# Every product of the two up layers as a pair of 64-row matmuls, with the inputs on both halves of the partitions

## The reference, cut to what matters

```python
x = attn_out.reshape(B * S, D)            # 8192 x 192: out[s] = sum_k w[head, k] * x[s - 6 + k]
g = x @ w_gate                            # 192 -> 1536
val = x @ w_val                           # 192 -> 1536
y = (g / (1 + exp(-g)) * val) @ w_out1    # 1536 -> 192
h = y @ w_in2                             # 192 -> 2048
a = where(h > 0, h, exp(min(h, 0)) - 1)
out = a @ w_out2                          # 2048 -> 192
```

## Time and profile before

| | |
|---|---|
| median of 2 runs | 1329.24 us (1328.96 to 1329.53) |
| profiled execution | 1330.26 us, span 1328.5 us |
| PE busy | 1314.7 us (99%), 6240 matmuls |
| DVE, ACT, POOL busy | 797.7, 667.7, 653.8 us |
| granted TensorE clock, mean | 0.997 |

### The profile page before, as it was taken

The page is one execution under the profiler, slowest core; times in us unless marked ns, Lnnn a source line. Parts: engine busy times, 40 slices in busy tenths (PEclk is TensorE's granted clock), DMA queues, the critical chain, the costliest instruction groups (busy, mean ns, idle before and its releaser), DMA issues.

```text
span 1328.5 us, 19686 instructions
## 1 busy us (share of the span) xinstructions
PE 1314.7 (99%) x6240; PEld 1036.9 (78%) x6240; DVE 797.7 (60%) x1196; ACT 667.7 (50%) x1104; POOL 653.8 (49%) x477
## 2 busy tenths in 40 slices
PE   7999999999999999999999999999999999999998
PEld 5768778687786877878788787877878778687787
DVE  7667466564665646557555675556656456564675
ACT  5455545454453644545455454554535545354454
POOL 5574445454454544545445454454544445454454
PEclk8999999999999999999999999999999999999999
DMA  8221000010010100101001010100001000010000
GB/s 186 54 74 25 13 9 16 12 24 12 8 17 11 24 12 8 28 0 24 12 11 24 0 24 12 22 13 8 16 12 24 12 8 16 12 24 12 8 13 13
DMA packets 93858, 28.15 MB, mean 21 GB/s; under 512 B 77456, under 2 KB 90256, under 8 KB 93840
## 3 DMA queue, kind: packets, MB, share of 16 engines
q1 hardware_dynamic: 93840, 27.93, 9.4%
HBM read 17.43 MB, written 6.29 MB: 18 GB/s over the span
## 4 chain that ended last, share of the span: by engine, by line
PE 96%; DVE 2%; issue 1%; ACT 0%; POOL 0%; POOLq 0%; DVEq 0%; ACTq 0%
PE up L769 55%; PE down L769 41%; DVE mixed L742 1%; DVE mixed L576 0%; DVE hidden L634 0%; ACT act L498 0%; DVE act L673 0%; DVE hidden L692 0%; DVE out_w L296 0%; ACT out_w L289 0%; DVE in_a_lo L582 0%; POOLq L67 0%; DVE hidden L735 0%; POOL hid_lo L384 0%; POOL head_of L368 0%
## 5 line engine op out<-in xcount | busy, mean ns | idle before, releaser
L384 POOL TENSOR_TENSOR hid_lo<-hidden,hid_hi 128x512 fp32r<-128x512 f32 x447 | 628.8, 1407 | 661.5 <-ACT hid_hi L480 387.0
L634 DVE TENSOR_TENSOR hidden<-act,up 128x512 f32<-128x512 f32 x192 | 131.8, 687 | 310.4 <-ACT act L467 307.2
L519 ACT ACTIVATE hid_hi<-hidden 128x512 fp32r<-128x512 f32 x256 | 162.0, 633 | 208.9 <-DVE hidden L692 208.9
L692 DVE SCALAR_TENSOR_TENSOR hidden<-act,up 128x512 f32<-128x512 f32 x256 | 175.7, 686 | 121.7 <-ACT act L498 117.3
L467 ACT ACTIVATE act<-up 128x512 f32<-128x512 f32 x192 | 114.7, 598 | 231.1 <-PE up L769 230.8
L769 PE MATMUL down<-out_w,hid_hi 128*128 128x384 f32 x1024 | 225.8, 342 | 0.3 <-DVE result L619 0.2
L673 DVE TENSOR_SCALAR act<-up 128x512 f32<-128x512 f32 x256 | 176.4, 689 | 63.2 <-PE up L769 57.9
L769 PEld LDWEIGHTS down<-out_w,hid_hi 128*128 128x128 f32 x1024 | 184.6, 188 | 28.5 <-issue 7.3
L480 ACT ACTIVATE hid_hi<-hidden 128x512 fp32r<-128x512 f32 x192 | 121.5, 633 | 162.2 <-PE down L769 91.2
L498 ACT ACTIVATE act<-act 128x512 f32<-128x512 f32 x256 | 161.2, 630 | 45.1 <-DVE act L673 39.0
L769 PE MATMUL down<-hid_hi,out_w 128*128 128x512 f32 x576 | 182.1, 424 | 0.0
(11 more groups left out here) (141 smaller groups left out, 1792.1 us busy)
## 6 DMA issues: line engine op xcount, KB each, us to landing
x_raw<-x_dram SPq DMA_DIRECT2D x144, 64.0 KB, 2.2
out_dram<-result SPq DMA_DIRECT2D x15, 384.0 KB, 2.6
swapped<-halves SPq DMA_DIRECT2D x32, 128.0 KB, 2.3
stage<-w_out_dram SPq DMA_DIRECT2D x7, 384.0 KB, 3.5
stage<-w_in_dram SPq DMA_DIRECT2D x4, 256.0 KB, 2.9
stage<-w_in_dram SPq DMA_DIRECT2D x8, 128.0 KB, 2.9
stage<-w_gate_dram SPq DMA_DIRECT2D x4, 192.0 KB, 4.2
stage<-w_val_dram SPq DMA_DIRECT2D x4, 192.0 KB, 4.6
```

The costliest lines, as they stand in the source:

```text
L384: return pool.tensor_tensor(hid_lo[:, slot, :], hidden[:, s, :], hid_hi[:, slot, :].bitcast(F32), ALU.subtract)
L519: nc.scalar.activation(hid_hi[:, k % RING, :], hidden[:, k % 2, :], ACT.Copy)\
L634: v.tensor_tensor(hidden[:, f % 2, :], act[:, f % 2, :], val_bank(f)[:, :], ALU.mult)\
L692: v.scalar_tensor_tensor(hidden[:, k % 2, :], act[:, k % 2, :], -1.0, elu_bank(n, k)[:, :], ALU.add, ALU.max).then_inc(elu_done, 1)
```

## The change

All up products of both layers are done as pairs of 64-row matmuls. The 192 channels are three groups of 64, and the weights of a group lie for two different blocks on the two halves: gate above and val below in the first layer, blocks 2j and 2j + 1 in the second. Nine pairs (three groups x three products) make two blocks. The data must lie on both halves: slot MAIN holds channels 0 to 63 above and 64 to 127 below, CROSSED the same with halves exchanged, written by DMA from MAIN, and TWICE the tail on both. In MAIN the upper half works on group 0 while the lower works on group 1, in CROSSED the other way round.

PE, DVE and ACT now walk the ELU phase by pairs j of blocks: two mins, then two ELUs; two exps, then two high parts. The down products there come in twos, four blocks behind (`LAG2`). Down products themselves are as they were. SP issues `cross1` and `cross2`, four DMAs of 128 KB for each chunk and layer. The tails' doubled weights go, and the weights come in other pieces.

```diff
-    LAG = 3
+    LAG, LAG2 = 3, 4
+    PAIR2 = N2 // 2
+    PARTS = 3
-    GROUPS = [(0, 3 * P), (3 * P, 9 * P), (9 * P, F1)]
+    GROUPS = [(0, P)] + [(f * P, (f + 2) * P) for f in range(1, N1 - 1, 2)] + [(F1 - P, F1)]
+        up1_w = {part: sb(f"up1_w_{part}", [P, PARTS, F1], F32R) for part in ("hi", "lo")}
+        up2_w = {part: sb(f"up2_w_{part}", [P, PARTS, F2 // 2], F32R) for part in ("hi", "lo")}
-        in_a = {k: sb(f"in_a_{k}", [P, T], F32R) for k in ("hi", "lo", "tail")}
+        in_a = {k: sb(f"in_a_{k}", [P, PARTS, T], F32R) for k in ("hi", "lo")}
+        MAIN, CROSSED, TWICE = range(PARTS)
-            return up[(k + is_int(n, CHUNKS)) % 3]
+            return (val_bank if k % 2 else gate_bank)(k // 2)
...
         @block.sync
+            def cross(data, hi_sem, lo_sem, count, crossed):
+                for part, made in (("hi", hi_sem), ("lo", lo_sem)):
+                    sp.wait_ge(made, count)
+                    for to, of in ((0, TAIL), (TAIL, 0)):
+                        sp.dma_start(data[part][to:to + TAIL, CROSSED, :].bitcast(F32),
+                                     data[part][of:of + TAIL, MAIN, :].bitcast(F32)).then_inc(crossed, 16)
+            def cross1(c):
+                cross(input1(c), in1_hi, in1_lo, 2 * c + 1, in1_crossed)
+            def cross2(m):
+                cross(input2(m), in2_hi, in2_lo, 2 * m + 1, in2_crossed)
             load_x(1, 1)
-            for i in range(AHEAD, PIECES1):
+            for i in range(AHEAD, PIECES1 - 1):
                 load_piece(i)
+            cross1(0)
+            load_piece(PIECES1 - 1)
...
             with sp.Fori(1, CHUNKS - 1) as n:
                 swap_halves(n)
                 load_x(n + 3, (n + 3) & (CHUNKS - 1))
+                cross1(n + 1)
                 store(n - 1)
+                cross2(n)
...
         @block.scalar, elu_phase
-                for k in range(N2):
-                    a.wait_ge(min_done, N2 * (n - 1) + k + 1)
-                    nc.scalar.activation(act[:, k % 2, :], act[:, k % 2, :], ACT.Exp).then_inc(exp_done, 1)
-                    if not is_int(n, CHUNKS):
-                        if k == 1:
+                for j in range(PAIR2):
+                    for k in (2 * j, 2 * j + 1):
+                        a.wait_ge(min_done, N2 * (n - 1) + k + 1)
+                        nc.scalar.activation(act[:, k % 2, :], act[:, k % 2, :], ACT.Exp).then_inc(exp_done, 1)
+                    for k in (2 * j, 2 * j + 1):
+                        if k == 2 and not last:
                             copy_main(n)
...
+                        if k == 2 and last:
+                            copy_halves(n - 2)
...
         @block.vector, elu_phase
+                for j in range(PAIR2):
+                    for k in (2 * j, 2 * j + 1):
...
+                        v.tensor_scalar(act[:, k % 2, :], elu_bank(k)[:, :], 0.0, None, ALU.min)\
+                            .then_inc(min_done, 1)
+                    if j == 1:
+                        if last:
+                            add_halves(n - 2)
+                        else:
+                            copy_tail(n)
...
         @block.tensor
-            def project_main(bank, w, data, f, lo_ready=None):
...
-            def project_lo_pair(f):
...
+            def project(upper, lower, w, j, data, part_ready=lambda slot: None):
                 c = slice(j * P, (j + 1) * P)
                 top, low = slice(0, TAIL), slice(TAIL, P)
+                for slot in (MAIN, TWICE, CROSSED):
+                    part_ready(slot)
+                    swapped = (1, 0, 2)[slot]
+                    for wpart, part in (("hi", "hi"), ("lo", "hi"), ("hi", "lo")):
+                        a = slot == MAIN and wpart == part
+                        z = slot == CROSSED and part == "lo"
+                        one = mm(upper[:, :], w[wpart][top, slot, c], data[part][top, slot, :], a, z)
+                        two = mm(lower[:, :], w[wpart][low, swapped, c], data[part][low, slot, :], a, z)
+                return one, two
...
             def mix_phase(n):
                 for f in range(N1):
                     if f < LAG:
                         if chunk1:
                             down1(0, N1 - LAG + f)
-                        elif not chunk0:
-                            down2(n - 2, N2 - LAG + f)
+                        elif not chunk0 and f < LAG2 // 2:
+                            down2(n - 2, N2 - LAG2 + 2 * f)
+                            down2(n - 2, N2 - LAG2 + 2 * f + 1)
...
             def elu_phase(n):
-                for k in range(N2):
+                for j in range(PAIR2):
...
+                    elif j >= LAG2 // 2:
+                        down2(n - 1, 2 * j - LAG2, down_free)
+                        down2(n - 1, 2 * j - LAG2 + 1)
...
                     else:
-                        down1(n, N1 - LAG + k)
+                        for f in ((N1 - 3, N1 - 2), (N1 - 1,))[j]:
+                            down1(n, f)
...
+                    even, odd = project(gate_bank(j), val_bank(j), up2_w, j, input2(n - 1), ready)
+                    even.then_inc(h2_ready, 1)
+                    odd.then_inc(h2_ready, 1)
```

## The result

The changed kernel takes **1398.87 us** (median; 1398.29 to 1399.44) against 1329.24 before: ratio 1.0524, 95% interval 1.0478 to 1.0569. It is slower, by 70 us; forecast were 1391 and +61. The span of the profiled execution grew from 1328.5 to 1397.7.

The account below looks back on a forecast made before the run. The prediction took PE's own instruction stream as the bound. Slots -32.8, round trips +48, lost excess -4, y_main waits +30, last phase +2, result waits +13 and start +5 summed to +61: 1391 us, range 1348 to 1445.

Parts of the forecast that it names:

- 140 slots less: PE, both layers: 12 fewer product slots in chunk 0, 8 fewer in each of 16 second-layer chunks, 0.234 us each: -32.8 us.
- the excess of -4: PE: full products behind 192-column ones lose a small excess, some 210 x 0.017 us: -4 us.
- y_main waits: ELU phase: PE's down product waits for copy_main, now behind exp 2 and exp 3; 2.0 us, 15 times: +30 us.
- the last phase's wait: Chunk 15: copy_halves moved like copy_main, so PE stalls alike for results: +2 us.
- result waits: Mix block 2, without a down product ahead: PE waits for add_halves' second result, 0.9 us, 14 times: +13 us.
- the start: Chunk 0: PE waits some 4 us for the crossed copies, possibly longer at half clock: +5 us, between 3 and 8.
- the fifth rival: PE's clock falls after each of 16 new stalls, some 3.3 us lost each: +53, 1444 us; chance 0.10.
- cheap pairs: Rival at the 2880 pairs: a product's fixed part vanishes beside its twin, pitch 0.22: -40, 1351 us; chance 0.14.
- dearer ones: Rival at the pairs: two loads and two issues in one slot add 5 to 17 ns: 1405 to 1440 us; chance 0.10.
- matmuls in turn: Rival at the pairs: the two halves don't run side by side: +674, 2065 us; chance 0.02.
- a misread order: Rival: copy and result waits don't come because the order was misread in the code: 1346 us; chance 0.05.
- bare loads: Rival at the 2880 pairs: a 0.105 us weight load per pair isn't covered: +302, 1693 us; chance 0.07.

Follow-up runs that it names:

- e4: The kernel before the change with its last 64-row pairs undone, so gate and val are five 128-row products each in every chunk: 1298.11 us.
- e5: e3 with the second down product of the ELU phase moved between the first three pairs and the other six, 95 more round trips: 1374.49 us.
- e7: e3 with the mix phase's down products four blocks behind and two at a time, 81 fewer round trips: 1305.74 us.
- e3: The changed kernel with the copy moves of both e1 and e2: 1338.51 us.
- e1: The changed kernel with copy_main and copy_tail (last ELU phase: copy_halves and add_halves) ahead of the second block pair's exps and mins: 1353.79 us.
- e2: The changed kernel with copy_halves and add_halves moved from mix block 1 to mix block 0: 1393.71 us.

## Why the prediction was right

It was right in sign and in each mechanism that it summed. That the size lies within 8 us is in part luck, as the terms show:

| step | forecast | shown |
|---|---|---|
| 140 slots less | -33 | counted, pitch of the pairs at 0.23 |
| a pair behind a pair | 0.234 | 0.232 to 0.233: some 3 to 6 us less in all |
| 123 more round trips at 0.39 | +48 | 0.41, 0.38, 0.40 in e4, e5, e7 |
| slots, trips and the excess of -4 together | +11 | 2 to 4: the loop has 0.16 a chunk in e3, the terms make 0.64 |
| y_main waits | +30 | 29.8 in 15 waits; gone in e1 |
| the last phase's wait | +2 | 2.7 |
| result waits | +13 | 13.0 in 14; gone in e2, e3 |
| the start | +5 | first down product at 34.98, before at 27.30: 8 with the slots saved |
| clock falls in the waits | not in the sum; a rival, +53 | about +12 |

**The step that was off is the clock**, which I kept out of the sum and gave to the fifth rival: "After each of 16 stalls: +53, 1444", with a chance of 0.10. It came true in part. Falls followed six of the 15 waits and the last phase's, and each of the six cost 1.6 us where the rival had 3.3; e1, which takes away the waits alone, takes away all of these falls. "The granted clock at 1.00 after the start", in my list of signs, was wrong.

The start was 3 us too low: the first low part ended at 19.83, not at 17.9, and SP issued the crosses from 22.42 on. The granted clock was at 0.50 from 16.1 to 32.6, half of that while PE waited; before it was so only from 17.2 to 23.6.

Against these 15 us stand 7 to 9 by which slots and round trips together came out cheaper than their terms. A pair pitch 1 to 2 ns shorter explains 3 to 6 of them; the rest is open. So two errors of opposite sign leave the 8 us between 1391 and 1399.

Two readings of mine need a word, though neither moves the time by more than 1 us. The 0.43 behind the lone pair isn't the way out alone, as it holds both the step behind a first pair and the way out: in a row of nine they lie apart, 0.34 and 0.33 instead of 0.234 each. And the sum, 1330.26 + 61.2 - 1.0, is 1390.5.

Of the other rivals: cheap pairs (0.22), dearer ones and matmuls in turn fall with the pitch, a misread order falls with the waits that came; bare loads fall with the PEld rows, where loads of both halves run under the pairs ahead. By one sentence of the Trainium skill, TensorE: Matmul & The Clock Gate, Part 3, they should overlap only across row groups; this trace contradicts it for 64-row loads (pitch 0.233) as the one before did for 128-row ones. Another sentence of the same part of the Trainium skill also lets a load run ahead when it targets the background weight buffer; that would fit both traces, though no row here shows such a buffer.

Why the idea could not win in this place: nine slots instead of ten save 0.234, and each entry into the form costs 0.4. Two ELU blocks lose 0.12 by it (4.76 against 4.64). Two mix blocks in one entry win 0.09 (6.94 against 7.03). The copies' order was a second and larger fault, independent of the idea: e3 takes back 60 of the 70 us without touching a single pair.

## What to carry to other kernels

Switching TensorE between 128-row and 64-row matmuls has a price per entry, here 0.4 us or 1.7 full products; pairs pay only where one entry saves more, so group them, and look for lone pairs to undo. When two items are made to arrive together, list every copy that stood between them on the other engines and ask what PE does next: a copy put behind the pair's own chain cost more (45 us, e1) than the whole change could bring (33 us of slots). Short regular stalls of PE can cost more in clock on top: here about 12 us on 45 of waits, and in e2 some 22 on 32.

## What the runs showed of the hardware

A wait of 2.0 us of PE, in the midst of dense work, was enough for a fall to the 1.2 GHz level, seen over 3.2 and 3.3 us in the windows above. It came behind six of 15 such waits in the changed kernel and behind 13 of 15 in e2, and behind none of the 14 waits of 0.93 in the changed kernel or in e1. A round trip from 128-row to 64-row matmuls and back cost 0.38 to 0.41 us (e4, e5, e7), with a weight load that starts only with its matmul at either switch. Pairs of 64-row matmuls with their two weight loads kept a pitch of 0.232 to 0.233 us, no longer than a full product's.
